# Scores of the next chunk at the head of the burst, in chunks 2 to 6 of a linear attention

## What is computed

```python
cur = einsum('bhd,bhe->bhde', u[None] * kt, vt)
y[:, :, t] = einsum('bhd,bhde->bhe', rt, state + cur)
state = w[None, :, :, None] * state + einsum('bhd,bhe->bhde', kt, vt)
```

## Time and profile before

| | us |
|---|---|
| median of 3 runs | 605.0 (604.84 to 605.68) |
| the profiled execution | 605.38 |
| its span, from first to last instruction | 603.6 |
| busy in it: TensorE | 598.4 |
| VectorE | 466.8 |
| ScalarE | 294.9 |
| GpSimd | 310.3 |

### The profile page before, as it was taken

One profiled execution on the slowest core, in us unless ns is written; L12 is line 12 of the kernel. 1 busy time (PEld: TensorE's weight loads), 2 busy tenths in 40 slices (PEclk: granted clock), 3 DMA queues, 4 the chain that ended last, 5 costly groups with the idle time before them and its releaser, 6 DMA issues.

```text
span 603.6 us, 10805 instructions
## 1 busy us (share of the span) xinstructions
PE 598.4 (99%) x3715; PEld 497.5 (82%) x3715; DVE 466.8 (77%) x751; ACT 294.9 (49%) x585; POOL 310.3 (51%) x371
## 2 busy tenths in 40 slices
PE   9999999999999999999999999999999999999998
PEld 6999987888788888888888888888887888888886
DVE  7888684374987877787787787788887887877895
ACT  4754433234444435335335335345776566556540
POOL 5663371785554746446446446426776745544100
PEclk9999999999999999999999999999999999999999
DMA  8765340002111110210010011100101110100004
GB/s 325 266 248 203 129 136 3 3 2 78 59 47 53 54 53 27 78 53 27 27 53 27 27 54 32 47 26 2 47 6 54 53 53 26 28 27 1 1 0 158
DMA packets 18316, 39.16 MB, mean 65 GB/s; under 512 B 2000, under 2 KB 10064, under 8 KB 18256
## 3 DMA queue, kind: packets, MB, share of 16 engines
q1 hardware_dynamic: 18256, 38.40, 18.9%
HBM read 36.01 MB, written 2.38 MB: 64 GB/s over the span
## 4 chain that ended last, share of the span: by engine, by line
PE 73%; DVE 1%; issue 0%; DVEq 0%
PE bank L2025 41%; PE bank L1975 30%; PE bank L1994 2%; DVE bank L1607 0%; DVE t_most L1605 0%; DVE bank L1640 0%; DVE w_lo L1650 0%; DVE acc L1627 0%; DVEq L1601 0%
## 5 line engine op out<-in xcount | busy, mean ns | idle before, releaser
L2025 PE MATMUL bank<-w_lo,w_hi 128*128 128x512 f32 (+1 forms) x735 | 186.0, 388 | 0.1
L1046 POOL TENSOR_TENSOR a_lo<-staging,a_hi 128x512 fp32r<-128x512 f32 (+3 forms) x96 | 97.7, 1027 | 149.6 <-ACT a_hi L1234 138.6
L2025 PEld LDWEIGHTS bank<-w_lo,w_hi 128*128 128x128 f32 x735 | 137.2, 188 | 29.0 <-DVE bank L1607 0.5
L1275 ACT ACTIVATE w_lo<-bank 128x512 fp32r<-128x512 f32 x81 | 48.2, 599 | 94.0 <-DVE bank L1640 62.6
L2025 PE MATMUL bank<-w_hi 128*128 128x512 f32 x351 | 91.8, 390 | 0.0
L1257 ACT ACTIVATE t_most<-bank 128x512 f32<-128x512 f32 x110 | 65.7, 597 | 52.4 <-PE bank L1975 51.5
L1620 DVE TENSOR_TENSOR acc<-bank,acc 128x512 f32<-128x512 f32 x86 | 58.8, 685 | 26.0 <-PE bank L2025 26.0
L2025 PEld LDWEIGHTS bank<-w_hi 128*128 128x128 f32 x351 | 65.8, 188 | 13.8 <-issue 0.2
L1607 DVE SCALAR_TENSOR_TENSOR bank<-bank,t_most 128x512 f32<-128x512 f32 x92 | 63.9, 695 | 15.0 <-PE bank L1975 12.4
L1975 PE MATMUL bank<-x_hi,a_hi 128*128 128x512 f32 x171 | 66.7, 390 | 0.3 <-DVE part L1607 0.3
L1975 PE MATMUL bank<-x_hi,a_lo 128*128 128x512 f32 x171 | 66.6, 390 | 0.0
(11 more groups left out here) (178 smaller groups left out, 1161.0 us busy)
## 6 DMA issues: line engine op xcount, KB each, us to landing
staging<-weights SPq DMA_DIRECT2D x40, 384.0 KB, 3.7
rkv_in<-rkv_n SPq DMA_DIRECT2D x10, 640.0 KB, 5.2
rk_in<-rk_t SPq DMA_DIRECT2D x12, 512.0 KB, 5.2
staging<-weights SPq DMA_DIRECT2D x4, 768.0 KB, 8.9
out<-acc SPq DMA_DIRECT2D x8, 256.0 KB, 2.0
p_bc<-p_normalised SPq DMA_DIRECT2D x2, 768.0 KB, 4.1
staging<-p_normalised SPq DMA_DIRECT2D x2, 768.0 KB, 4.8
rkv_in<-rkv_n SPq DMA_DIRECT2D x2, 448.0 KB, 5.7
```

Of the source, the lines that this page charges most:

```text
L1046: pool.tensor_tensor(new, src, high.bitcast(F32), ALU.subtract).then_inc(sem["alo"], 1)
L1275: act.activation(tile_hi[number % H_RING], over_bank(q, pos), ACT.Copy).then_inc(sem["thi"], 1)
L2025: last = pe.matmul(bank[:, home, cols], v_parts[a][q % 2][:, f * DM + k * P:f * DM + (k + 1) * P], tiles[c][number % H_RING][:, cols], sta ...
```

## The change

In the bursts of chunks 2 to 6 attend(i+1) is issued first, ahead of key_values(i) and values(i); from chunk 7 on it stays behind them, as it is in all bursts before. No instruction, wait or buffer is added or removed, and the lists of the other engines are not touched.

```diff
--- before.py
+++ after.py
@@ -1858,10 +1858,14 @@
                     elif what == "attend":
                         attend(i)
                     elif what == "burst":
+
+                        scores_first = ALONE <= i < KV_LATE - 1
+                        if scores_first:
+                            attend(i + 1)
                         if i > 1:
                             key_values(i)
                         values(i)
-                        if ALONE <= i < CH - 1:
+                        if ALONE <= i < CH - 1 and not scores_first:
                             attend(i + 1)
                     elif what == "hidden":
                         hidden(i)
```

## The result

| | before | after |
|---|---|---|
| median, us | 605.07 (6 runs, 604.84 to 605.68) | 609.52 (6 runs, 607.38 to 610.09) |
| after / before | | 1.0063 (95% interval 1.0053 to 1.0073) |
| the profiled execution | 605.38 | 609.53 |
| its span | 603.6 | 607.8 |
| mean granted clock of TensorE in it | 1.000 | 0.997 |

The change costs 4.45 us where 1.5 were forecast. The sign was right, the size was not, and the time lies outside the range of 605.6 to 608.2. The six executions fall into two groups: 607.38 and 607.76 us with a mean granted clock of 1.000, and 609.51 to 610.09 us with 0.997. The profiled one is of the second group.

A forecast was written before the change was run, and what follows sets the result against it. TensorE, busy 598.4 of 603.6 us, was taken as the bound. The terms 0.7 + 0.2 + 0.35 + 0.2 + 0.1 = 1.55, say 1.5 us, on 605.0 gave 606.5 us, range 605.6 to 608.2.

The forecast's parts named there:

- What bounds the kernel, and that a new wait goes to the end: Whole kernel: TensorE busy 598.4 of 603.6 us, so new waits in bursts 2 to 6 lengthen it almost in full.
- The burst itself: Bursts 4 to 6: a hidden step followed by scores costs +0.1 us for all three together.
- Term 1: Burst 2: scores wait for chunk 2's second mask, +0.85 less 0.17 absorbed later, +0.7 us (0.6 to 0.9).
- Term 2: Head of burst 3: scores wait for chunk 4's scaled keys, undisturbed by GpSimd, +0.2 us (0 to 1.6).
- rival (b): Burst 3: GpSimd's products still disturb the scaling of chunk 4's keys, wait 1.4 us, 607.8 us in all; chance 0.12.
- the forecast's chance: Whole kernel: the prediction's main case, 606.5 us with its own range 606.0 to 607.2, was given 0.45.
- Term 3: Burst 4: later carry(4) delays VectorE's evictions, holding the second tile of output(8), +0.35 us (0 to 0.7).
- Term 4: Burst 6: VectorE's later train delays chunk 6's masks, so attend(7) waits, +0.2 us (0 to 1.0).
- Burst 7: Burst 7, in its old order: carry(6) comes later but just in time, 0, at most +0.3 us.
- (a): Only burst 2 pays; burst 3 is free and bursts 4 to 6 nearly so, 605.7 us; chance 0.27.
- (c): VectorE's train breaks, delaying low parts for output(9) and output(10) and chunk 6's masks: 607.5 us; chance 0.13.
- (d): The order gains: each burst 0.2 us shorter and no wait in burst 2, 604.0 us; chance 0.03.

The follow-up runs named there:

- the filled kernel: Changed kernel with VectorE's scaling of chunk 4 made always late, plus 32 unused bf16 matmuls ahead of burst 3's scores: 609.41 us, ratio 1.0068.

## Why the prediction was wrong, by its own steps

- *What bounds the kernel, and that a new wait goes to the end.* Right. The 0.45 us that burst 10 took back in one profile of the changed kernel stayed away in the other. That such a thing could happen was to be read from the earlier trace rows: a wait of 0.67 us behind the changed bursts.
- *The burst itself.* The new order costs nothing of its own: 3.09 us from the scores to the output step in the filled kernel, as in the earlier trace rows. The 0.1 us for the transitions are 0.
- *Term 1, burst 2.* Forecast +0.7, measured +0.84 - 0.24 = +0.6: the wait, its releaser and what was absorbed were right.
- *Term 2, burst 3.* This is the step that failed. Forecast +0.2, measured +1.99, beyond its upper bound of 1.6. The mechanism, scaling against GpSimd, was right; its size hung on the sentence "the products begin at some 33.95", which moved the landing by as much as the issue. They began at 32.66. The time from the load's issue (L756, first line below) to the start of the products was 32.04 - 25.79 = 6.25 us before, 5.0 after, and 4.85 to 6.3 in the other traces: one execution's latency was taken for a constant, where by rival (b) 0.6 us decided. A second, smaller slip: the masks of chunk 3 ended at 33.08, not 32.8, as the split ahead of them took 1.06 us, with GpSimd beside it, instead of the 0.55 of the kernel before (second line). Rival (b) was this case, at 0.12; it had no term for the clock, and its 607.8 is what the changed kernel took when its clock held (606.8 to 608.0). It deserved at least the forecast's chance.

```profile
25.79 0.75 SPq L756 DMA_DIRECT2D rkv_in<-rkv_n  x1
...
30.64 0.55 DVE L1373 TENSOR_TENSOR w_lo<-staging,w_hi 128x384 fp32r<-128x384 f32 x1
```

- *The granted clock.* No term, and no rival: this is the second step that failed. The prediction gives no reason for putting it at nothing. The longest wait of its own sum was 1.0 us, but rival (b) had one of 1.4 and its price left the clock out too. It is worth 1.62 us in the profiled execution, and carries the time out of the range. How far out is in part chance: the clock fell in four of the first six executions, and in one of five when the kernel ran again, where the median, 2.7 us over the kernel before, lies inside the range.
- *Term 3, the evictions.* Forecast +0.35, measured +0.29. *Term 4, masks of chunk 6.* Forecast +0.2, measured +0.27. Both by the wait that was named. Burst 7 lost nothing.
- *Rivals.* (a) did not come: burst 3 was not free in any profile of the changed kernel, and even with the overlap taken away by a wait it cost some 0.75 us. (c) did not happen, its chains held. (d) had nothing for it.

What stays open: why the products can start 4.85 us after the load's issue in one execution and 6.3 in another; why the clock fell at 37.2 us in one profiled execution, 1.5 us behind the start of the scores, and at 35.6 in another, 0.1 us behind it, with waits of 1.93 and 1.77 us; and whether the length of the wait alone decides that it falls, since no execution of the changed kernel with its clock held was profiled.

## What to carry to other kernels

Before an instruction is moved to the head of a group, compare when its operands are ready with the head's time, not with its old place: the work that used to stand in front of it was cover for them. A step that waits on a DMA's landing and leans on an overlap with another engine has two prices, not one; if the gap between them is under a microsecond, give both near equal chances, and let the range reach over the dearer. And when a new idle stretch of TensorE comes near 2 us, price what follows at the lower clock too.

## What the runs showed of the hardware

- In two profiled executions a wait of 1.77 and of 1.93 us on a TensorE that was otherwise 99% busy was followed by half the granted clock for 3 to 4 us, at a cost of about 1.6 us; waits of up to 1.42 us were not. Behind a longer wait (3.01 us in the profile) it fell in four executions of four; 32 bf16 matmuls in that wait (1.96 us) kept it up in five of five.
- The same 512-column `tensor_tensor` with two SBUF inputs took 0.68 us with GpSimd idle and 1.10 to 1.50 us behind a GpSimd operation that had begun before it. Begun 0.02 us ahead of that one (scores first in burst 2 alone) it took 0.67 us, and GpSimd's operation 1.52 instead of 1.02. Four small operations of VectorE took 4.1 to 5.1 us in all beside a row of GpSimd sums instead of 1.0.
- A 640 KB load, issued with three others, let its user start 4.85 to 6.3 us after its issue, in kernels that issue it alike.
